# Seven products of quarters in place of eight in the up projections of a fused attention and expert kernel, batch by batch

## What is computed

```python
# attention: batch 2, 8 heads, 768 positions, head size 64, window of 96 keys and 8 global keys
a = softmax(scale * q @ k.T + bias, masked);  x = (a @ v) as [1536, 512]
p = domain_probs / (domain_probs.sum(-1, keepdims=True) + 1e-09)
for e in range(4):
    h = np.maximum(x @ w1[e], 0.0)          # [1536, 1024]
    out += p[:, e:e + 1] * (h @ w2[e])      # [1536, 512]
a = out @ w1_gated;  b = out @ w2_gated     # [1536, 1024] each
y = ((a * b) @ w3) @ w_out                  # [1536, 512]
```

## Time and profile before

| | before |
|---|---|
| median of three runs | 893.7 us |
| profiled execution | 897.0 us |
| its span, first to last instruction | 895.1 us |
| TensorE matmul busy | 864.2 us |
| dense stages, first matmul 157.55 us to the end | 737.6 us |

### The profile page before, as it was taken

How to read it: one execution, slowest core, us unless ns; L and a number is a source line. 1 busy time by engine, 2 the same in 40 slices (tenths; PEclk the granted TensorE clock), 3 DMA queues, 4 the chain that set the end, 5 groups by cost and what they waited for, 6 DMA issues and landing times.

```text
span 895.1 us, 13994 instructions
## 1 busy us (share of the span) xinstructions
PE 864.2 (97%) x5062; PEld 815.9 (91%) x5062; DVE 225.4 (25%) x589; ACT 240.3 (27%) x550; POOL 341.1 (38%) x317
## 2 busy tenths in 40 slices
PE   7889975999999999999999999999999999999998
PEld 6657643999999999999999999999999999999897
DVE  7355674111211211210210210220321211111111
ACT  3456674301114201114200113210224421112020
POOL 3545475622328512328412338411329431202020
PEclk9999999899999999999999999999999999999999
DMA  9453552210003100004100004100004100000000
GB/s 336 159 215 126 183 201 104 95 47 0 0 0 123 64 0 0 0 0 138 50 0 0 0 0 141 47 0 0 0 0 141 49 12 23 0 35 0 35 0 35
DMA packets 12713, 52.79 MB, mean 59 GB/s; under 512 B 1920, under 2 KB 1936, under 8 KB 9744
## 3 DMA queue, kind: packets, MB, share of 16 engines
q1 hardware_dynamic: 11472, 50.36, 15.7%
q10 hardware_dynamic: 1152, 2.10, 0.6%
q0 software_dynamic: 64, 0.03, 0.0%
HBM read 47.21 MB, written 5.27 MB: 59 GB/s over the span
## 4 chain that ended last, share of the span: by engine, by line
PE 88%; DVE 4%; POOL 3%; DMA 2%; issue 1%; ACT 1%; SPq 0%; ACTq 0%; DVEq 0%; POOLq 0%
PE bank L52 28%; PE bank L54 28%; PE bank L53 28%; POOL pr L453 2%; PE bank L540 1%; PE bank L530 1%; PE bank L557 1%; DMA k<-k 1%; DVE pt L517 1%; DVE pr L491 1%; DMA fold_mt_raw<-m3t 1%; POOL fold_mt_l L203 1%; DVE den L502 0%; DVE fold_wo_l L198 0%; DVE bias_tmp L378 0%
## 5 line engine op out<-in xcount | busy, mean ns | idle before, releaser
L895 POOL TENSOR_TENSOR hl<-hf,hh 128x384 fp32r<-128x384 f32 x128 | 129.8, 1015 | 307.0 <-ACT hh L837 307.0
L52 PE MATMUL bank<-xh,w1h 128*128 x640 | 215.2, 336 | 5.4 <-issue 5.4
L54 PE MATMUL bank<-xh,w1l 128*128 x640 | 214.9, 336 | 0.0
L53 PE MATMUL bank<-xl,w1h 128*128 x640 | 214.9, 336 | 0.0
L52 PE MATMUL bank<-hh,w2h 128*128 128x384 f32 x512 | 171.0, 334 | 0.0
L53 PE MATMUL bank<-hl,w2h 128*128 128x384 f32 x512 | 171.0, 334 | 0.0
L54 PE MATMUL bank<-hh,w2l 128*128 128x384 f32 x512 | 171.0, 334 | 0.0
L837 ACT ACTIVATE hh<-hf 128x384 fp32r<-128x384 f32 x128 | 67.2, 526 | 331.4 <-DVE hf L950 331.4
L52 PEld LDWEIGHTS bank<-xh,w1h 128*128 128x128 f32 x640 | 121.1, 189 | 5.8 <-issue 5.7
L53 PEld LDWEIGHTS bank<-xl,w1h 128*128 128x128 f32 x640 | 121.1, 189 | 0.1
L54 PEld LDWEIGHTS bank<-xh,w1l 128*128 128x128 f32 x640 | 121.0, 189 | 0.0
(11 more groups left out here) (92 smaller groups left out, 943.9 us busy)
## 6 DMA issues: line engine op xcount, KB each, us to landing
raw<-weights SPq DMA_DIRECT2D x20, 1024.0 KB, 4.8
k<-k SPq DMA_DIRECT2D x8, 704.0 KB, 8.8
v<-v SPq DMA_DIRECT2D x8, 704.0 KB, 5.2
fold_mt_raw<-m3t SPq DMA_DIRECT2D x7, 512.0 KB, 8.1
q<-q SPq DMA_DIRECT2D x8, 384.0 KB, 6.6
gate<-gates SPq DMA_DIRECT2D x1, 3072.0 KB, 12.4
out<-raw SPq DMA_DIRECT2D x12, 256.0 KB, 2.0
fold_wo_raw<-m_out SPq DMA_DIRECT2D x8, 256.0 KB, 7.3
```

What stands on the lines that cost most here:

```text
L52: nc.tensor.matmul(out, wh, xh, start=start, stop=False)
L53: nc.tensor.matmul(out, wh, xl, start=False, stop=False)
L54: return nc.tensor.matmul(out, wl, xh, start=False, stop=stop)
L895: nc.gpsimd.tensor_tensor(hl[:, c], hf[f % HF][:, :], hh[:, c].bitcast(F32), ALU.subtract).then_inc(h_low, 1)
```

## The change

The three up projections (`x @ w1` of an expert, and the two of the gated stage) are computed by Strassen's scheme in Winograd's form. The inner dimension of 512, the outputs and the tokens of a batch are halved. Seven products of quarters replace eight: P1 = A11 B11, P2 = A12 B21, P3 = S4 B22, P4 = A22 T4, P5 = S1 T1, P6 = S2 T2, P7 = S3 T3, with sums S of weight quarters and T of token quarters. A group `i` makes four results C11, C12, C21, C22 of 128 by 384 each from 42 matmuls (7 products, 2 blocks of k, 3 matmuls); before, 48 made them. There are 4 groups for an expert and a batch, 8 for the gated stage and a batch. Here A are weights, B tokens.

The sums S (four operations of 128 by 256) are made by VectorE for each group (`up_sums`). ScalarE makes the high parts of 128 by 768 and 128 by 1024 (`up_high`) and GpSimd the low parts of the same sizes (`up_sums_low`, `up_raw_low`). The sums T (128 by 768) are made and split once for a batch and stage. Since two products add in one bank and its contents are needed between them, VectorE and ScalarE read the bank in between: ScalarE copies P1 (`snap`), VectorE makes u2 = P6 + P1, u3 = P7 added to that, C22 = u3 + P5, C21 after P4, C12 = u2 + P3. TensorE's product 2 waits for `snapped`, 7 for `u2_made`, 4 for `u3_made`, 3 for `c22_made`. VectorE also makes the low parts of the hidden units (`h_split_low`), which GpSimd made before.

The dense stages now run batch by batch: four experts and the gated stage for tokens 0 to 767, then all of it again for the rest. Weights are loaded and split in both rounds. The gate is applied after `h @ w2` (`drain`: a product with the gate, then an addition). Loops over experts and tiles are written out. The seven token splits of the first batch stand in attention turns 12 to 18, the weights of groups 0 and 1 in turns 19 to 22. ScalarE and VectorE no longer split the attention's output; VectorE copies it.

```diff
-TT = 384
-NT = TOK // TT
+TT = S // 2
...
+    def up_sums(self, dve, g):
...
+        if g:
+            dve.wait_ge(self.a_sum_low, g)
+        nc.vector.tensor_tensor(s1, a21, a22, ALU.add).then_inc(self.a_step, 1)
+        dve.wait_ge(self.a_step, 4 * g + 1)
+        nc.vector.tensor_tensor(s2, s1, a11, ALU.subtract).then_inc(self.a_step, 1)
+        nc.vector.tensor_tensor(a21, a11, a21, ALU.subtract).then_inc(self.a_step, 1)
+        dve.wait_ge(self.a_step, 4 * g + 3)
+        nc.vector.tensor_tensor(s4, a12, s2, ALU.subtract).then_inc(self.a_step, 1)
...
+    def product(self, pe, i, bank, a, b, start, done):
...
+        for k in range(2):
+            w = slice(a * QUART + k * P, a * QUART + (k + 1) * P)
+            x = slice((2 * b + k) * TT, (2 * b + k + 1) * TT)
+            last = hi_lo_products(nc, self.bank[bank][:, 0:TT], (self.ah[s][:, w], self.al[s][:, w]),
+                                  (self.bh[:, x], self.bl[:, x]), start and k == 0, k == 1, adds_on=True)
+        last.then_inc(done, 1)
...
+    def product2(self, pe, i):
+        pe.wait_ge(self.snapped, i + 1)
+        self.product(pe, i, self.banks(i)[0], A12, B21, False, self.p2)
...
+    def product7(self, pe, i):
+        pe.wait_ge(self.u2_made, i + 1)
+        self.product(pe, i, self.banks(i)[1], S3, T3, False, self.p7)
...
+    def product4(self, pe, i):
+        pe.wait_ge(self.u3_made, i + 1)
+        self.product(pe, i, self.banks(i)[1], A22, T4, False, self.p4)
...
+    def product3(self, pe, i):
+        pe.wait_ge(self.c22_made, i + 1)
+        self.product(pe, i, self.banks(i)[2], S4, B22, False, self.p3)
...
+    def expert(self, pe, n):
+        i0 = UPS * (n // E) + 4 * (n % E)
+        self.product1(pe, i0)
+        for i in range(i0, i0 + 4):
+            if i > i0:
+                self.product4(pe, i - 1)
+                self.product3(pe, i - 1)
+            self.product6(pe, i)
+            self.product5(pe, i)
+            self.product2(pe, i)
+            self.product7(pe, i)
+            if i < i0 + 3:
+                self.product1(pe, i + 1)
...
+        self.down(pe, n, 0, 0, range(KD))
+        self.product4(pe, i0 + 3)
+        self.product3(pe, i0 + 3)
+        for k in self.ORDER[1:]:
+            self.down(pe, n, 0, k, range(KD))
...
+    def gated(self, pe, t):
+        i0 = UPS * t + 4 * E
+        self.product1(pe, i0)
+        self.product2(pe, i0)
+        self.product5(pe, i0)
...
+        if e == E - 1:
+            self.b_split_high(act, T1, 2 * t + 1)
+            self.b_split_high(act, T2, 2 * t + 1)
+            act.wait_ge(self.x2_made, self.x2_count(t) + 8)
+            self.b_split_high(act, B22, 2 * t + 1)
+            self.b_split_high(act, T3, 2 * t + 1)
+            self.b_split_high(act, T4, 2 * t + 1)
...
+    def group_tail(self, dve, i):
+        self.add_u3_c22(dve, i)
+        self.add_c21(dve, i)
+        self.h_split_low(dve, i, 22)
+        self.add_c12(dve, i, self.c_of(12))
+        self.h_split_low(dve, i, 21)
...
+    def expert_vector(self, dve, n):
...
+            if g:
+                self.group_tail(dve, i0 + g - 1)
+            self.add_u2(dve, i0 + g)
+            if g:
+                self.h_split_low(dve, i0 + g - 1, 12)
+            if g == 0 and n == 0:
+                self.up_sums(dve, 2)
+            self.h_split_low(dve, i0 + g, 11)
+            if g == 1:
+                self.up_sums(dve, i0 + 3)
+            if g == 3:
+                self.up_sums(dve, i0 + 4)
...
+        if e == E - 1:
+            dve.wait_ge(self.x2_made, self.x2_count(t) + 8)
+            self.sum_t2(dve, s)
+            self.sum_t3(dve, s)
+            self.b_split_low(dve, self.nc.vector, T2, s)
+            self.sum_t4(dve, s)
+            self.b_split_low(dve, self.nc.vector, T3, s)
...
+            if f:
+                self.gated_tail(dve, t, f - 1)
+            self.add_u2(dve, i)
+            if f:
+                self.gated_low(dve, t, f - 1)
+            if 1 <= f and i + 2 < B * UPS:
+                self.up_sums(dve, i + 2)
...
+                    if folded_by <= c < folded_by + OPS:
+                        dense.b_split_low(pool, nc.gpsimd, SPLITS[c - folded_by], 0)
+                    if c in (folded_by + OPS, folded_by + OPS + 2):
+                        dense.up_sums_low(pool, (c - folded_by - OPS) // 2)
...
-                pe.wait_ge(windows.x_low, UNITS // PER_OUT)
```

More of the change, by code:

```diff
@@ L12 @@
+import functools
 from contextlib import ExitStack
@@ L40 @@
 PIECE = DM
-HALF = 4 * PIECE
 SCALE = 1.0 / D ** 0.5
@@ L482, in scalar, with outputs, store @@
             nc.scalar.activation(self.pt[0][:, 0:w], self.ps_t[0][:, 0:w], ACT.Copy).then_inc(self.even_copied, 1)
+    def outputs(self, dve, g):
+        dve.wait_ge(self.attended, (g + 1) * PER_OUT)
+        if g < OUTS0:
+            start = g * PER_OUT
+            while start < (g + 1) * PER_OUT:
+                end = min(start // 3 * 3 + 3, (g + 1) * PER_OUT)
+                hp, i = divmod(start, UPP)
+                to = x_block(hp, i // 3) + i % 3 * P
+                last = self.nc.vector.tensor_copy(self.x0[:, to:to + (end - start) * P],
+                                                  self.ps_o[:, start % PER_OUT * P:(start % PER_OUT + end - start) * P])
+                start = end
+        else:
+            if g >= OUTS0 + 2:
+                dve.wait_ge(self.x_stored[g % 2], 16 * ((g - OUTS0) // 2))
+            last = self.nc.vector.tensor_copy(self.x_stage[g % 2][:, :], self.ps_o[:, :])
+        last.then_inc(self.x_out, 1)
+    def store(self, sp, g):
+        sp.wait_ge(self.x_out, g + 1)
+        sp.dma_start(self.x_dram[:, (g - OUTS0) * PER_OUT * P:(g - OUTS0 + 1) * PER_OUT * P],
+                     self.x_stage[g % 2][:, :]).then_inc(self.x_stored[g % 2], 16)
     def bias_and_max(self, dve, u):
-        w, r, head = self.width(u), u % 2 * 2, u // UPP // 2 * 2
+        w, r, head = self.width(u), u % 2 * 2, u // UPP % KD * 2
         table = self.setup.bias_w if u % UPP else self.setup.bias_0
@@ L1065, in build @@
         attn_done = sem("attn_done")
-        end = nc.sbuf_usable_end
-        area = Area(lay["acc"], end)
-        fold = Fold(nc, sem, lay, area, bank, m3t.rearrange("(f p) n -> f p n", p=P), m_out, folded)
-        setup = Setup(nc, sem, area, n_both, gate_in, gates)
-        windows = WindowAttention(nc, sem, Area(area.at, end), bank, setup, q2, k2, v2, xh, xl)
-        full = FullAttention(nc, sem, Area(setup.tables_at, end), bank, setup, q2, k2, v2, xh, xl)
-        dense = dense_stages(nc, sem, lay, bank, weights, folded, gates, out, xh, xl, fold, setup.g_stored, attn_done)
+        x_stored = [sem(f"x_stored{s}") for s in range(2)]
+        low = Area(lay["hh"], lay["x_stage"])
+        high = Area(lay["parts"], end)
+        fold = Fold(nc, sem, lay, low, bank, m3t.rearrange("(f p) n -> f p n", p=P), m_out, folded)
+        setup = Setup(nc, sem, low, n_both, gate_in, gates)
+        cells = Area(setup.cells_at, lay["x_stage"])
+        dense = Dense(nc, sem, lay, bank, weights, folded, gates, x_dram, x_stored, out, fold, setup.g_stored)
+        x_stage = [nc.alloc_sbuf_tensor_at(f"x_stage{s}", [P, PER_OUT * P], F32, offset=lay["x_stage"] + 2 * KB * s)
+                   for s in range(2)]
+        windows = WindowAttention(nc, sem, low, cells, high, bank, setup, q2, k2, v2, dense.x, x_stage, x_dram, x_stored)
+        full = FullAttention(nc, sem, Area(setup.tables_at, end), bank, setup, q2, k2, v2, dense.x, x_dram, x_stored)
         block = ctx.enter_context(nc.Block())
@@ L1091, in _ @@
                 dense.first_loads(sp)
+                dense.gate_load(sp, 0)
                 for seg in range(2, SEGS):
                     windows.load(sp, seg)
-                dense.gate_load(sp)
+                    if seg >= 5:
+                        windows.store(sp, OUTS0 + seg - 5)
+                for g in range(OUTS0 + 3, OUTS):
+                    windows.store(sp, g)
             with sp.Else():
@@ L1123, in _ @@
                 full.scalar(act)
-                for p in range(EARLY):
-                    dense.weight_high(act, 0, p, first=True)
+                act.wait_ge(full.x_moved, 1)
+                for b in SPLITS:
+                    dense.b_split_high(act, b, 0)
+                for g in range(2):
+                    dense.up_high(act, g)
             dense.scalar(act)
@@ L1145, in _ @@
                 full.gpsimd(pool)
-                for p in range(EARLY):
-                    dense.weight_low(pool, 0, p)
+                for b in SPLITS:
+                    dense.b_split_low(pool, nc.gpsimd, b, 0)
+                for g in range(2):
+                    dense.up_low(pool, g)
             dense.gpsimd(pool)
@@ L1175, in _ @@
                 full.vector(dve)
-            nc.vector.memset(setup.scratch[:, 7:8], 0.0).then_inc(attn_done, 1)
-            dve.wait_ge(attn_done, 1)
+                dense.sum_t1(dve)
+                dense.sum_t2(dve, 0)
```

(5 more changed lines are left out.)

1010 lines of the change are left out of this document (681 added, 329 removed).

## The result

The changed kernel takes 949.99 us (median of 4 runs, 949.44 to 951.57), the kernel before 893.81 (893.14 to 896.13) beside it: a ratio of 1.063, 95% interval 1.060 to 1.065. It is 56 us slower with 288 matmuls less. The profiled execution took 950.47 us (span 948.3) against 897.0 (895.1), so the traces differ by 53.2 us of span.

The account below looks back on a forecast made before the run. TensorE was taken to bound the dense stages, its matmuls busy 97% of the span. Terms -49.7 + 36 + 38 + 21 + 15 - 2 = +58 on 893.7 gave 952 us; forecast 935 to 975 (chance 0.55), range 880 to 985.

Parts of the forecast that it names:

- Matmuls: Up projections on TensorE: 288 matmuls fewer at 0.1727 us each, -49.7 us.
- Experts: Expert stage: TensorE waits for u3 behind the sums and for late u2, 4.0 us per expert, +36 in all.
- the lock: VectorE operations with two SBUF operands and GpSimd ones reading SBUF exclude each other; priced at 54 us in dense stages.
- the order's share: Experts: sums standing before u3 in groups 1 and 3 stall TensorE 1.95 us per expert, even without the lock.
- Gated groups: Gated stage: VectorE's list has no slack for the lock; groups run 4.0 or 1.5 us over 7.25, +38 together.
- Change of stages: From experts to gated stage, twice: P1's copy queued behind T splits idles TensorE and lowers its clock, +21 us.
- Attention and start: Attention turns lengthened by GpSimd's low parts and waits, +15; start of the dense stages, -2; together +13 us.
- term 6: Start of the dense stages: TensorE needn't wait for L508, but 4.1 us without an engine as cause stay; -2 us.
- the longer queue: Attention: GpSimd's B low parts (6.4) and the low parts in turns 19 to 22 (4.1) lengthen its turns, 10.5 us.
- the waits of `den` and the sums: Attention: T sums and two `up_sums` wait for GpSimd and then stand ahead of `den`, 6.7 us.
- Rival (a): Whole kernel: no lock felt, operations with two SBUF operands don't collide or rarely meet; 888 us, chance 0.14.
- Rival (d): Experts, gated groups and attention: the lock costs half the forecast's price; 920 us, chance 0.15.

Follow-up runs that it names:

- runs 4 and 5: Changed kernel with GpSimd's dense-stage weight low parts as two memsets each (4), or made on 32 columns only from the second expert (5): 903.8 and 905.2 us.
- Run 7: Changed kernel with GpSimd's low parts of the first batch's B operands and first two w1 groups as one memset each, without reads: 933.9 us.
- run 2: Changed kernel with the weight sums of expert groups 1 and 3 moved behind u3 and C22: 959.7 us, ratio 1.073.
- Run 10: Changed kernel with memsets for GpSimd's low parts of w1, w2 and first B operands, and P1's copy ahead of T1 to T4's splits: 883.7 us.
- run 1: Changed kernel with ScalarE's copy of P1 of the first gated group moved ahead of the splits of B22, T3 and T4: 941.7 us, ratio 1.053.

## Why the prediction was right

It said 952 us and 950.0 was measured. By its own terms:

- **Matmuls**: -49.7 predicted. 5062 - 4774 = 288 less, the spacing 0.172 us in a stretch without a stop.
- **Experts**: +36 predicted, +35 measured. Eight times 4.07, and 2.7 more in the first, whose stops are 1.30, 2.58, 0.41, 0.76 and 0.10 instead of 1.42, 0.41, 0.76 and 0.10. The parts were right too: without the lock (runs 4 and 5) an expert is 2.0 us above 62.2, the order's share (1.95 predicted), the lock the other 2.0. Where the stall shows was a little off: u2 of group 2 comes only 0.4 us late, not 1.6; the u3 of the same group, not in the prediction, stops TensorE for 0.76; and u3 of group 3 for 0.10, not 0.45.
- **Gated groups**: +38 predicted, +33 measured (stops of the first batch 15.9 with their 0.16 us of spacing each, of the second 12.7; the other 5 were matmuls at the lower clock around three of the stops of 2.7 us, for example 34 in 7.34 us at 880 to 890, and the stop that followed was shorter by as much). The period was 10.9 and 8.8, not 11.3 and 8.8. The lock costs more at the second sum (2.47) than forecast, and less at the second product, which just missed the low part in the group shown (0.56 us) and took 1.97 in the next. The prediction's list of VectorE's work in a group is 9 x 0.6 + 1.6 = 7.0 us, not the 7.3 that it states; runs 4 and 5 agree that it fits into 7.25.
- **Change of stages**: +21 predicted, +19 measured: two gaps of 7.3 (6.1 to 7.9 forecast) and 1.8 and 2.1 for the clock, less than the 2.7 each. The 10.5 us taken for each lay at the upper end of the prediction's own 8.8 to 10.6.
- **Attention and start**: +13 predicted, +14.2 measured (157.55 to 171.79). TensorE's idle time just ahead of that first matmul fell from 5.43 to 3.19 us, the -2 of term 6; for the 3.19 that stay the trace names no engine as the cause. Run 7 shows GpSimd's low parts as the cause of all or most of attention's part; how much of that is the longer queue (10.5 predicted) and how much the waits of `den` and the sums (6.7), no run tells apart. Of one thing the prediction said nothing: the granted clock in attention's late turns fell, 0.74 at 130 to 150 against 1.00 before. It isn't what sets the turns: the dense start at 171.8 came with a clock of 0.77 at 120 to 150, the one at 175.5 (run 2) with 0.89, and runs 7 and 10 say the same.

Together -49.7 + 35 + 33 + 19 + 14.2 = 51.5 of the 53.2 us between the spans; 1.7 aren't assigned. The mechanism and its sizes held, but that the time came within 2 us is in part luck: by its terms the prediction was +58 and the spans differ by 53.2. The profile of the kernel before lay 3 us above its median and that of the changed one only 0.5, so between the medians it is +56.2.

One reading of the prediction is a little off: behind 27.17 only 4.55 us are left of GpSimd's 9.11, less than two times 2.40, so its operation got in slightly before VectorE was done. Nothing in the sum hangs on it.

Rival (a), no lock, would have been 888; runs 4 and 5 with the lock taken away in the dense stages gave 904 and 905, in the main since attention kept its part: the start was 14.5 and 13.4 us later than before, where the rival has 6.5. Rival (d), half the price, would have been 920. In the dense stages the prediction priced the lock at 54 us (36 - 18.6 and 38 - 1), and taking GpSimd's reads away gave back 46.

What stays open: a version that keeps the computation and gains from the seven products. Run 10 bounds what freeing VectorE from GpSimd's reads and the early copy can give, 10 us below the kernel before. To run plain products in the gated stage, whose 33 us stand against 16.6 of matmuls saved, wasn't tried.

## What to carry to other kernels

A trade of TensorE work for elementwise work is priced on the engines that take it: here 50 us of matmuls were bought with 3.1 us per group of VectorE operations whose two operands lie in SBUF, beside GpSimd operations of 4 to 7 us that read SBUF, and in the dense stages alone the pair's waits (46 us) took nearly all of it back, before the queue orders and attention came on top. Count, per group and in order, which VectorE operations read two SBUF operands and where a GpSimd read can get in between two dependent ones; moving or cutting them shifts such a wait from one result to the next as long as the list is full. And look at what stands in a queue ahead of the small copy that the next stage waits for: that was 19 us, and moving one call gave back 12.6 of it in the stage itself (run 1).
